# Turning every unit from 4 on by quarter products, and moving five loads on SyncE's queue, in a Fourier filter followed by two MLPs

## The reference

```
X = rfft(x, axis=1)
y = irfft(X * (filt_r + 1j*filt_i), n=3008, axis=1)
x = y.reshape(6016, 256)
h = x @ w_in;  g = maximum(0.01*h, h);  x = g @ w_out          # d_ff = 2048
h = x @ w_in2; r = maximum(h, 0); out = (r*r) @ w_out2
```

## Time and profile before

| | us |
|---|---|
| median of 3 runs | 1063.06 (1062.47 to 1063.35) |
| the profiled execution, its own time | 1064.17 |
| its span | 1062.0 |
| TensorE busy | 1056.9 |
| VectorE busy | 831.8 |
| ScalarE busy | 561.7 |
| GpSimd busy | 320.2 |

### The profile page before, as it was taken

How to read it: one execution, slowest core, us unless ns; L and a number is a source line. 1 busy time by engine, 2 the same in 40 slices (tenths; PEclk the granted TensorE clock), 3 DMA queues, 4 the chain that set the end, 5 groups by cost and what they waited for, 6 DMA issues and landing times.

```text
span 1062.0 us, 14667 instructions
## 1 busy us (share of the span) xinstructions
PE 1056.9 (100%) x5456; PEld 881.0 (83%) x5456; DVE 831.8 (78%) x1142; ACT 561.7 (53%) x979; POOL 320.2 (30%) x287
## 2 busy tenths in 40 slices
PE   9999999999999999999999999999999999999998
PEld 9559888888888888888998888888888888888998
DVE  2878998887887887787887886887887887786666
ACT  3666665554554655555554554544554554454543
POOL 1895764434343343341221211220220220210000
PEclk9999999999999999999999999999999999999999
DMA  9786000122112112112344000100100100100100
GB/s 313 213 280 222 10 1 18 35 53 49 49 51 48 52 48 51 52 34 54 120 152 145 21 1 1 40 1 1 40 1 1 40 1 1 40 0 1 40 1 35
DMA packets 66727, 61.48 MB, mean 58 GB/s; under 512 B 40689, under 2 KB 53857, under 8 KB 66657
## 3 DMA queue, kind: packets, MB, share of 16 engines
q1 hardware_dynamic: 66160, 60.06, 18.3%
q10 hardware_dynamic: 496, 0.49, 0.1%
HBM read 36.55 MB, written 23.99 MB: 57 GB/s over the span
## 4 chain that ended last, share of the span: by engine, by line
PE 98%; DMA 1%; DVE 0%; POOL 0%; ACT 0%; issue 0%; SPq 0%; DVEq 0%; ACTq 0%
PE PS L1092 16%; PE PS L1091 16%; PE PS L1090 16%; PE PS L1098 14%; PE PS L1100 14%; PE PS L1099 14%; PE PS L1064 2%; PE PS L964 2%; PE PS L1044 1%; PE PS L1021 1%; PE PS L991 1%; DMA X<-in_x 1%; PE PS L1000 1%; DVE GF L905 0%; POOL AF L465 0%
## 5 line engine op out<-in xcount | busy, mean ns | idle before, releaser
L709 ACT ACTIVATE GH<-GF 128x512 fp32r<-128x512 f32 (+1 forms) x384 | 238.7, 622 | 298.6 <-DVE GF L907 154.3
L913 DVE TENSOR_TENSOR GL<-GF,GH 128x512 fp32r<-128x512 f32 (+1 forms) x384 | 272.1, 712 | 109.4 <-ACT GH L709 102.6
L1092 PE MATMUL PS<-GH,WOL 128*128 128x512 f32 (+1 forms) x768 | 295.8, 385 | 0.0
L1090 PE MATMUL PS<-GH,WOH 128*128 128x512 f32 (+1 forms) x768 | 295.8, 385 | 0.0
L1091 PE MATMUL PS<-GL,WOH 128*128 128x512 f32 (+1 forms) x768 | 295.8, 385 | 0.0
L1098 PE MATMUL PS<-XH,WIH 128*128 128x512 f32 (+1 forms) x672 | 259.7, 386 | 0.3 <-ACT SN L687 0.3
L1100 PE MATMUL PS<-XH,WIL 128*128 128x512 f32 (+1 forms) x672 | 258.8, 385 | 0.0
L905 DVE SCALAR_TENSOR_TENSOR GF<-GF 128x512 f32<-128x512 f32 (+1 forms) x192 | 172.8, 940 | 1.6
L1091 PEld LDWEIGHTS PS<-GL,WOH 128*128 128x128 f32 x768 | 144.2, 188 | 27.0
L1092 PEld LDWEIGHTS PS<-GH,WOL 128*128 128x128 f32 x768 | 144.2, 188 | 26.8
L1090 PEld LDWEIGHTS PS<-GH,WOH 128*128 128x128 f32 x768 | 144.2, 188 | 26.7
(11 more groups left out here) (92 smaller groups left out, 948.4 us busy)
## 6 DMA issues: line engine op xcount, KB each, us to landing
V<-zu SPq DMA_DIRECT2D x12, 512.0 KB, 7.0
zu<-U SPq DMA_DIRECT2D x31, 192.0 KB, 3.7
out_y<-YT SPq DMA_DIRECT2D x5, 1024.0 KB, 4.3
X<-in_x SPq DMA_DIRECT2D x8, 512.0 KB, 9.5
wi<-PWH SPq DMA_DIRECT2D x16, 224.0 KB, 2.5
wi<-PWL SPq DMA_DIRECT2D x16, 224.0 KB, 3.1
WIH<-wi SPq DMA_DIRECT2D x8, 448.0 KB, 3.6
WIL<-wi SPq DMA_DIRECT2D x8, 448.0 KB, 4.4
```

Of the source, the lines that this page charges most:

```text
L709: nc.scalar.activation(GH[:, g, 0:width(s)], GF[:, g, 0:width(s)], ACT.Copy).then_inc(g_hi[kind], 1)
L913: nc.vector.tensor_tensor(GL[:, g, 0:w], GF[:, g, 0:w], GH[:, g, 0:w].bitcast(f32), ALU.subtract).then_inc(g_lo[kind], 1)
L1090: nc.tensor.matmul(acc, wh, xh, start=first, stop=False)
L1092: return nc.tensor.matmul(acc, wl, xh, start=False, stop=last)
```

## The change

All units from 4 on are turned by quarter products; before, only the even ones were. Units 0 to 3 keep the full turn, so the odd units 5, 7, 9, 11, 13 and 15 change. On SyncE's queue, the loads of weight chunks 5 and 6 move from iterations 1 and 2 to iterations 5 and 6. The pieces of V's first half are read one in each of iterations 8, 9, 10 and 11, and pieces 4 and 5 in iteration 11 as well; before, two were read in each of iterations 8, 9 and 10.

```diff
         def by_quarters(i):
 
-            return i >= 4 and i % 2 == 0
+            return i >= 4
...
                 if 9 + i < UNITS:
                     load_filter(9 + i)
-                if i in (1, 2):
-                    load_w1i(4 + i)
+                if i in (5, 6):
+                    load_w1i(i)
                 if i == NU:
                     for n in range(NU - STORES, NU):
                         sp.wait_ge(*stored(n))
-                if 0 <= i - NU < MH // 8:
-                    load_v(0, 2 * (i - NU))
-                    load_v(0, 2 * (i - NU) + 1)
+                if NU <= i < NU + 4:
+                    load_v(0, i - NU)
+                if i == NU + 3:
+                    load_v(0, 4)
+                    load_v(0, 5)
```

## The result

The changed kernel takes 1065.35 us (median of 19 runs, 1063.3 to 1070.67); the kernel before takes 1063.35 us in runs beside it (19 runs, 1062.47 to 1064.8). The ratio is 1.0024, 95% interval 1.0014 to 1.0034. I had forecast 1062.4 us, with 1061.4 to 1063.8 as the range: a small gain, and it is a loss of 2.0 us. The runs also spread over 7.4 us where those of before spread over 2.3.

A forecast was written before the change was run, and what follows sets the result against it. TensorE's pace through the filter, nearly matched by a three-engine loop, was taken as the bound. Turns gave 0.84 us, V's queue left 0.70: profiled 1064.17 to 1063.47, median 1063.06 to 1062.4 us, range 1061.4 to 1063.8.

The forecast's parts named there:

- What bounds the kernel: Filter: TensorE's own work and a three-engine loop nearly coincide; at the filter's end V came with under 0.1 us to spare.
- Six turns: Odd units' turns from 5 on: quarter turns bring unit 15's inverse 0.84 us sooner, bounds nothing to 1.7 us.
- the walk: Filter iterations stepped forward with timings from the trace: unit 15's inverse at 75.75 us, 76.59 for the kernel before.
- the loop allows 2.75 us a unit: Filter loop through TensorE, VectorE and GpSimd with quarter turns: 8.24 us for three units, 2.75 a unit.
- The rule of the Trainium skill on small products: Turns: about 60 cycles on top of each matmul; one after another, six turns cost some 14 us more; trace disagreed.
- The waits of a quarter turn: Quarter turn waiting for both ScalarE copies of the unit before: costs nothing, with 0.2 us of cover.
- Weight chunks 5 and 6: Two 256 KB loads moved to iterations 5 and 6: nothing; without room, up to 0.7 us of transfer each.
- V's first half: Moved reads on the DMA queue: pieces not late; V's second half comes 0.55 to 0.84 us sooner, 0.70 taken.
- rival 2: Filter's end: burst of three V reads delays the last stores, +0.5 to +1.8 us, 1063.6 to 1064.9; chance 0.15.
- a faster V: Filter's end: V's second half comes 0.70 us sooner, the middle of 0.55 and 0.84.
- no change within 0.2%: Whole kernel: time stays within 0.2% (2.1 us) of before, chance 0.96, each side 0.02.

The follow-up runs named there:

- run 1: Changed kernel's quarter turns in every unit from 4 on, against the kernel before, all loads left where they stood before: 1065.81 us, ratio 1.0030.
- run 3: Changed kernel without the seven filter loads from unit 9 on (units 9 to 15 reuse filters of units 0 to 6): 1064.5 us, ratio to before 1.0015.
- run 5: Changed kernel with 16 small products ahead of everything, adding 64 instructions to TensorE's program: 1068.64 us (4 runs).
- run 10: As run 3, with weight chunks 5 and 6 and pieces 2 to 5 of V's first half issued behind unit 12's stores: 1071.2 us.
- run 9: Changed kernel with 8 small products ahead of everything, adding 32 instructions; executed once, no time given.
- run 6: Kernel before, its loads unmoved, with quarter turns in units 4, 5, 6, 8, 9, 11, 12, 14, 15 and full turns in 7, 10, 13: 1063.16 us, ratio 0.9999.
- run 2: Changed kernel's moved loads only, odd units keeping the full turn as in the kernel before: 1064.04 us, ratio 1.0007.
- run 4: Changed kernel's loads, but units from 4 on turned by 16 products 128 rows deep, half the instructions of a quarter turn: 1074.7 us.
- run 8: Kernel before with only weight chunks 5 and 6 moved to units 5 and 6: 1063.55 us, ratio 1.0000.
- run 7: Kernel before with only V's first half read as in the changed kernel: 1064.63 us, ratio 1.0008.
- run 11: Kernel before with the same 16 small products ahead as run 5: 1068.61 us over six runs, three near 1066.4 and three near 1070.4.

## Why the prediction was wrong

**What bounds the kernel** stood: TensorE's pace through the filter, and the end of the filter with V just in time.

**Six turns, 0.84 us.** The mechanism was right as far as it went. Where no hold disturbs, from unit 4's turn to unit 9's, the changed kernel takes 13.50 us and run 1 13.47, before 13.87: 0.37 to 0.40 gained, and the walk, done over with the prediction's constants, gives 0.37. From unit 4's turn to unit 15's the changed kernel takes 33.57 us; without the 3.20 of holds that is 30.37, and the walk had 30.29 (65.93 - 35.64). In the same way runs 1, 3, 5 and 10 show 0.61 to 0.83 us gained at unit 15's turn, against the walk's 0.74; run 9, with four holds in it, shows none. At unit 15's inverse the gain under the holds is 0.82 us against 0.84, but that this agrees so closely is partly luck: run 1 has 0.66 there and run 5 has 0.39. For run 6's turns the same walk gives about 0.3 us at unit 15's inverse, and the run shows none.

**The step that failed is the one that lists what a quarter turn costs.** I priced its columns and its two waits. I did not price its 128 instructions as instructions, though both counts were there to read: 64 records against 8, and a program of 2 x 5456. Against "the loop allows 2.75 us a unit" stands a supply of 256 instructions in 4.3 to 6.4 us, which is the time from one boundary to the next wherever the next one held. TensorE goes on again at 50.12, 55.45 and 60.54 us in the changed kernel, one block apart: 5.33 and 5.09 us. In run 1 the last two restarts (64.25 and 69.92) are 5.67 apart. TensorE uses a block up in 3.5 to 5.0 us there (from one restart to the next hold). Before, a pair of units needs about 213 instructions in 5.6 us, so a block lasts 6.7 us on average and never ran out; with nine turns of twelve it still did not (run 6). The margin was small: in the profiled execution of before, one packet started 4.03 us behind its boundary (48.51 against 44.48) and ended 2.1 us ahead of the next, where the holds end 1.3 to 1.5 us behind a packet.

That the holds stand at block ends is shown by every one of them: the changed kernel and runs 1, 3, 5, 9 and 10 have 18 holds at boundaries, of 0.10 to 2.10 us, and each stands at a record whose number is the same (193) modulo 256, with the program moved (runs 5 and 9) or not. Behind each of the 18, TensorE goes on 1.27 to 1.48 us after an instruction packet's end. That it takes the turns and not the loads is shown by runs 1 and 2.

A refill has three parts in these traces. In the kernels with twelve quarter turns one packet starts between each two boundaries of the filter. (In run 4 two packets start 0.9 and 1.7 us ahead of the boundary, so the fetching can run somewhat ahead of what TensorE's records show.) Ahead of the 18 holds it starts 1.3 to 3.9 us behind the boundary, the packet takes 0.9 to 1.7 us, and TensorE goes on 1.3 to 1.5 us after it. So what varies most is how late the packet starts. That this is so *because* the DMA engines are busy is only partly shown. For it speak run 3, where the packets started 1.0 to 1.7 us sooner without the filter loads, and the stretch from about 35 to 38 us, in which the DMA share is 0.07 to 0.22 and the packets of the changed kernel and of runs 1, 3, 5, 6, 9 and 10 start 0.6 to 1.8 us behind. But the order is not that of the share: a packet started 1.26 us behind its boundary at a share of 0.92 (60.54 in the changed kernel) and one 3.03 us behind at the same share (50.12). What makes the one late and the other not stays open. And as a dense block is used up in as little as 3.5 us, the slower of the refills in the quiet stretch (1.8 + 1.4 + 1.3 us, an estimate from run 1's packet there) would have made a hold too.

**The rule of the Trainium skill on small products** ("TensorEngine Tiling (Array Packing)", "Instruction Overhead") pointed the right way, but its reason, about 60 cycles for each matmul, is not what cost here: the unbroken quarter turns keep their 0.90 us. The page of the Trainium skill that I should have read is "Runtime: NRT & Kernel Launch", section "Instruction fetch mechanics": instructions come in blocks of 16 KiB, 256 instructions, and crossing a block is "mostly hidden". The traces agree with the size of the block (16.3 KB, holds 256 records apart) and not with the second part: up to 2.10 us at one crossing.

**The spread.** Four of the 19 runs of the changed kernel have a granted clock of 0.995 to 0.998 over the whole span, and they are the ones of 1067.2 to 1070.7 us; the other 15 have 1.000 and 1063.3 to 1066.8. Run 3's profile shows such an execution: a hold of 1.88 us, then 10 us at half clock. Run 10's has 3.4 us at half clock behind its hold of 1.86 us. Run 1's has none behind its 2.10 us. So the holds can cost twice: once in themselves, and again by the clock, in some executions. That this happened in the four runs above is inferred from their clocks; none of them was profiled.

**The waits of a quarter turn** cost nothing on TensorE that shows, as priced. **Weight chunks 5 and 6** cost nothing (run 8). **V's first half:** rival 2, the burst that delays the last stores, was right in kind. With before's turns it costs about 1.2 us by the medians (run 7; interval 0 to 1.8), and the +0.5 to +1.8 named holds that, though the interval reaches down to nothing. I gave it 0.15 and took a faster V instead; the assumption that failed is that the queue works through the same data in the same time. The changed kernel doesn't pay for it on top, since its turns are later than the reads: its profile has 3.9 us from the last store (79.94) to V's reads (83.80), and TensorE went on with V 9.66 us behind its last inverse, no later than before.

The rival that I lacked is the supply of instructions; my chances (0.96 for no change within 0.2%) had no room for it.

No version beat the kernel before. Run 6 equals it within 0.1%.

## What to carry to other kernels

Count instructions, not only columns: where a rewrite splits one product into many small ones, compare the instructions per microsecond of the densest few microseconds with what the program's own stream has been seen to deliver, here 256 in 4.3 to 6.4 us beside busy transfers. A hold in the middle of a run of like instructions, with no wait in it and "issue" as releaser, at places a fixed number of instructions apart, is that stream running dry. The DMA view settles it: look for an instruction packet that ends shortly ahead of each restart. Mixing dense and sparse units, as the kernel before does, keeps the average below the limit: here nine dense turns of twelve cost nothing, and twelve cost 2 us.

## What the runs showed of the hardware that was not expected

- TensorE's instructions come in packets of 16.3 KB on a queue of their own, one for each 256 instructions (43 packets for 10912, 46 for 11584), and TensorE stood up to 2.10 us for one.
- In the filter of the kernels with twelve quarter turns, each instruction packet started only behind the boundary before the one it was needed at, 0.6 to 3.9 us behind it; at the 18 holds TensorE went on 1.27 to 1.48 us after the packet's end.
- A hold of 1.88 us was followed by about 10 us at a granted clock of 0.50, though TensorE was at work again; one of 1.86 us by about 3.4 us (run 10), and one of 2.10 us by none (run 1).
- 32 records of 128 rows by 48 columns of weights, with 128 columns of data, stand 0.06 us apart (1.9 us in all); 64 records of 64 by 48, with 64 columns of data, stand 0.014 us apart (0.90 in all).
- 16 products of no use at the start made the time 1068.6 us in place of 1063.5 (run 11, six runs in two groups near 1066.4 and 1070.4), more than the 2.6 us by which unit 4's turn came later.
